# Early dense weights loaded sooner and rounded later, another order of the first loads and of TensorE's step

## The chip, the cores and the metric

The kernel runs on one core of one Trainium2 chip. The metric is the device time of one execution in microseconds (us), as the median of several runs.

## What is computed

Attention with buckets, and two dense blocks behind it. There are 2 x 8 heads of 768 positions and 64 features. A query sees a key only if six projected signs of both agree.

```python
mask = q_bucket[:, :, :, None] == k_bucket[:, :, None, :]
scores = np.where(mask, scale * q @ k.T, -1e9)
attn = softmax(scores)                       # over 768 keys
x = (attn @ v) gathered to 1536 x 512
h = x @ w_in;  g = P(h) / Q(h);  x = g @ w_out          # 512 -> 2048 -> 512
h = x @ w_in;  g = h * clip(h + 3, 0, 6) / 6;  out = g @ w_out
```

## The kernel before

Each engine has its own instruction stream, written out by hand with semaphores between them. The attention stage runs over 8 pairs of heads (`PAIRS`). A head has 6 tiles of 128 queries, so a pair has 12 steps, and tile n is number 12 i + j. I write "step 7" for j = 7. Step j of a pair contains, on each engine and in this order:

- TensorE (`step`, line 863): the scores of tile n into one of two banks; the turning (transposing) of the probabilities of tile n - 3, in two halves, by six transposes; in odd steps a third of a weighing of values by the probabilities of the pair before (`weigh`, line 824); at j = 1 the projection of the next pair (`project`). The scores of tile n wait for the exponential of tile n - 2 (line 808), since both use one bank. In the last pair the weighings stand at steps 1, 2, 4, 6, 8 and 9.
- VectorE (line 637): the maximum of tile n, the inverse of the row sum of n - 1, its copy of the turned second half of n - 3; at j = 2 the threshold that makes the bit rows of the next pair (line 595), at t = 1 of a head (t counts the tiles of a head) the lower halves of the head after next (line 603). The threshold writes the one tile `bits`, so it waits until the last head's bit rows have been moved out of it (line 599).
- GpSimd (line 404): scale and bias of tile n, the normalising of tile n - 1, and, a step behind ScalarE, the lower part of early weights.
- ScalarE (`step`, line 471): a copy of the weighed values at a head's start, the exponential of tile n - 1, at a head's start the upper halves of the head after next (`split_hi`), its copy of the turned first half of n - 3 (`take_turned`), and, in steps `EARLY_AT` of pairs 3 to 6, the rounding of one half of a dense weight slot (`split_weights`).

SyncE asks for nearly all DMAs, in one queue written by hand: raw heads, values, the moves that place keys and bit rows of a head in other partitions (`place_head`, line 289, with four waits inside it) and the weights (`load_weights`, line 301). In pairs 3 to 6 (`EARLY_PAIR`, four of them) it loads one dense slot each, w_in and w_out, 256 KB each, through the two buffers `w_raw`; a buffer is free again when GpSimd has subtracted from it.

Head 0 is loaded twice: straight into `raw[0][0]`, and with queries and keys exchanged into `raw[1][0]`, the tile that pair 1's first head needs next. Behind the attention stage the two dense blocks run over 3 chunks of 512 tokens and 16 slots each.

Of the kernel before, what the change touches and what calls it, by code (L numbers as in the profile page):

```python
# [24 lines left out]
ACT = mybir.ActivationFunctionType  # L25
AX = mybir.AxisListType

P = 128
# [5 lines left out]
def bucket_attention_and_two_mlps(nc, q, k, v, proj, w_in0, w_out0, poly_a, poly_b, w_in1, w_out1, out):  # L34
# [19 lines left out]
    TURN_LAG = 3  # L54
# [6 lines left out]

    EARLY_SLOTS = 4
    EARLY_PAIR = PAIRS - 1 - EARLY_SLOTS
    EARLY_AT = (4, 8)

    QC = 1.0 + 1e-6
    assert DM == HEADS * D and 2 * D == P and CHUNK == BANK and TILES == 6 and KT == 4
# [6 lines left out]
    def dram_head(i, u):  # L74
        return (i % BATCH) * HEADS + (i // BATCH) * 2 + u
# [15 lines left out]
    with ctx:  # L91
        def sb(name, shape, dt=F32, stack=ctx):
            return stack.enter_context(nc.sbuf_tensor(name, shape, dt))
# [33 lines left out]
        with attn:  # L127
            raw = [[sb(f"raw{e}{u}", [P, SEQ], F32, attn) for u in range(2)] for e in range(2)]
            pt_first = [[None, None], [None, None]]
            for g in range(2):  # L130
                pt_first[0][g] = sb(f"pt_first0{g}", [P, TILES, HALF], F32, attn)
            q_cross, k_cross, q_main, k_main = zip(*[
                [sb(f"{name}{u}", [P, SEQ], F32R, attn) for name in ("q_cross", "k_cross", "q_main", "k_main")]
                for u in range(SETS)])
            bits = sb("bits", [P, HALF], F32R, attn)
            v_nat = [[sb(f"v_nat{e}{u}", [P, TILES, D], F32, attn) for u in range(2)] for e in range(2)]
            probs = [sb(f"probs{j}", [P, SEQ], F32, attn) for j in range(4)]
            for g in range(2):
                pt_first[1][g] = sb(f"pt_first1{g}", [P, TILES, HALF], F32, attn)
            pt_second = [sb(f"pt_second{g}", [P, TILES, HALF], F32, attn) for g in range(2)]  # L140
            attn.pop_all().close()
        t_abs = [sb(f"t_abs{j}", [P, CHUNK]) for j in range(2)]
        t_den = [sb(f"t_den{j}", [P, CHUNK]) for j in range(2)]
# [112 lines left out]
        @block.sync  # L256
        def _(sp):
            def load_raw(i, u):
                to = raw[i % 2][u]
                sp.dma_start(to[0:D, :], q_dram[dram_head(i, u), :, :]).then_inc(raw_in[i % 2][u], 16)  # L260
                sp.dma_start(to[D:P, :], k_dram[dram_head(i, u), :, :]).then_inc(raw_in[i % 2][u], 16)

            def load_v(i):
                if i >= 2:
                    sp.wait_ge(pv_done, 2 * (i - 1))
                for u in range(2):
                    sp.dma_start(v_nat[i % 2][u][:, :, :].rearrange("p t d -> p (t d)"),
                                 v_dram[dram_head(i, u), :, :]).then_inc(v_in[i % 2], 16)

            def move(dst, src):  # L270
                return sp.dma_start(dst.bitcast(F32), src.bitcast(F32))

            def place_keys(h):

                c = h % SETS
                sp.wait_ge(hi_made, h + 1)
                move(k_main[c][0:D, :], q_main[c][D:P, :]).then_inc(moved_in[c], 16)
                move(k_cross[c][0:D, :], q_main[c][D:P, :]).then_inc(moved_in[c], 16)

            def place_bits(queue, h, side):  # L280

                c, at = h % SETS, 2 * QUAD * (h % 2) + MASKROWS * side
                to = (q_main, k_main)[side][c]
                for half in range(2):
                    cols = slice(HALF * half, HALF * (half + 1))
                    rows = slice(at + QUAD * half, at + QUAD * half + MASKROWS)
                    queue.dma_start(to[D:KROWS, cols].bitcast(F32), bits[rows, :].bitcast(F32)).then_inc(main_in[c], 16)  # L287

            def place_head(h):

                c = h % SETS
                place_keys(h)
                sp.wait_ge(bits_made, h // 2 + 2)
                place_bits(sp, h, 1)
                sp.wait_ge(lo_made, h + 1)
                move(k_cross[c][D:P, :], q_cross[c][D:P, :]).then_inc(moved_in[c], 16)
                sp.wait_ge(moved_in[c], moved(h))
                move(q_cross[c][D:P, :], q_main[c][0:D, :]).then_inc(main_in[c], 16)
                place_bits(sp, h, 0)

            def load_weights(m, f):

                at = FT * m + f
                for j, src in enumerate((w_in_dram[m][:, :, P * f:P * (f + 1)], w_out_dram[m][:, f, :])):
                    after(sp, w_lo_made, 2 * at - 1 + j)
                    dst = w_raw[j][:, :]
                    if j == 0:
                        dst = dst.rearrange("p (c n) -> p c n", c=KT)
                    sp.dma_start(dst, src).then_inc(w_in_sem[j], 16)

            sp.dma_start(raw[0][0][0:D, :], q_dram[dram_head(0, 0), :, :]).then_inc(raw_in[0][0], 16)
            sp.dma_start(raw[1][0][D:P, :], q_dram[dram_head(0, 0), :, :]).then_inc(swapped_in, 16)
            sp.dma_start(proj_raw[D:P, :], proj).then_inc(proj_in, 16)
            load_raw(0, 1)
            sp.wait_ge(bits_made, 1)
            sp.wait_ge(first_q, 2)
            place_bits(sp, 0, 0)
            load_v(0)
            place_head(1)
            sp.wait_ge(first_k, 2)  # L320
            load_raw(1, 0)
            load_raw(1, 1)
            load_raw(2, 0)
            load_raw(2, 1)
            sp.dma_start(a_col[:, :], poly_a.partition_broadcast(P)).then_inc(poly_in, 16)
            sp.dma_start(b_raw[:, :], poly_b.partition_broadcast(P)).then_inc(poly_in, 16)

            for h in range(NHEAD):
                i, u = divmod(h, 2)
                if u == 0 and i >= 1:  # L330
                    load_v(i)
                if h + 2 < NHEAD:
                    place_head(h + 2)
                if h + 6 < NHEAD:
                    load_raw((h + 6) // 2, h % 2)
                if u == 0 and EARLY_PAIR <= i < EARLY_PAIR + EARLY_SLOTS:
                    load_weights(0, i - EARLY_PAIR)
            for f in range(EARLY_SLOTS, FT):
                load_weights(0, f)
            for f in range(FT):  # L340
                load_weights(1, f)

            def store(c):

                for j in range(4):
                    sp.wait_ge(y_free, 4 * (CHUNKS + c) + 4 + j + 1)
                    tile = 4 * c + j
                    sp.dma_start(out_dram[tile // TILES, tile % TILES, :, :],
                                 (t_den + t_num)[j][:, :]).then_inc(stored[j], 16)

            for c in range(CHUNKS):
                store(c)
            for j in range(4):
                sp.wait_ge(stored[j], 16 * CHUNKS)
# [65 lines left out]
        @block.scalar  # L420
        def _(act):

            act.dma_start(raw[0][0][D:P, :], k_dram[dram_head(0, 0), :, :]).then_inc(raw_in[0][0], 16)
            act.dma_start(proj_raw[0:D, :], proj).then_inc(proj_in, 16)
            act.dma_start(raw[1][0][0:D, :], k_dram[dram_head(0, 0), :, :]).then_inc(swapped_in, 16)
            act.wait_ge(sel_made, 4)
            for c in range(2):
                act.dma_start(bit_col[:, c:c + 1], bit_row[0:1, c, :]).then_inc(bit_col_in, 16)
# [58 lines left out]

            act.wait_ge(swapped_in, 32)
            for to in (k_main, k_cross):
                nc.scalar.activation(to[0][0:D, :], raw[1][0][0:D, :], ACT.Copy).then_inc(first_k, 1)  # L490
            act.wait_ge(bits_made, 1)
            for half in range(2):
                cols, rows = slice(HALF * half, HALF * (half + 1)), QUAD * half + MASKROWS
# [92 lines left out]
        def _(dve):  # L586
# [72 lines left out]
            dve.wait_ge(bit_col_in, 32)  # L659
            threshold(0, slice(0, D), first=True)  # L660
            dve.wait_ge(swapped_in, 32)
            nc.vector.tensor_copy(q_cross[0][D:P, :], raw[1][0][D:P, :]).then_inc(first_q, 1)
            nc.vector.tensor_tensor(q_cross[0][0:D, :], raw[0][0][0:D, :], q_main[0][0:D, :].bitcast(F32),
                                    ALU.subtract).then_inc(first_q, 1)
            dve.wait_ge(first_q, 4)
# [117 lines left out]
        def _(pe):  # L783
# [79 lines left out]
            def step(i, j):  # L863
                u, t = divmod(j, TILES)
                h, n = 2 * i + u, 2 * TILES * i + j
                scores(h, i, u, n, j, t)
                if n >= TURN_LAG:
                    for half in range(2):
                        turn_probs(n - TURN_LAG, half)
                if i == PAIRS - 1 and j in LAST_WEIGH:  # L870
                    weigh(i - 1, *LAST_WEIGH[j])
                if 1 <= i < PAIRS - 1 and t in WEIGH_AT:
                    weigh(i - 1, u, WEIGH_AT[t])
                if j == PROJECT_AT and i + 1 < PAIRS:
                    project(i + 1, 0)
                    project(i + 1, 1)

            project(0, 0)
            project(0, 1)
# [87 lines left out]
```

## Time and profile before

| | |
|---|---|
| median of 3 runs | 822.86 us (822.78 to 823.11) |
| profiled execution | 823.14 us, its span 821.3 us |
| TensorE busy | 766.7 us, 93% of the span |
| VectorE, ScalarE, GpSimd busy | 479.0, 439.6, 223.3 us |
| the eight pairs' first scores at | 13.96, 49.85, 79.37, 108.38, 146.12, 183.85, 218.92, 255.36 us |
| dense blocks | from about 301 us to the end |
| moves of 192 KB between partitions, issue to landing | 2.6 us (keys and their lower halves) |

The span is the time from the first to the last instruction that the profile shows; the profiled execution's own time lies around it. A busy TensorE is not one at its peak: the length of a matmul in the rows is modelled and overlaps its neighbour's, so the distance from one start to the next is what counts. The granted clock (PEclk) is 1.00 at 2.4 GHz and 0.50 at 1.2 GHz; a mean between them is a mixture of the two.

### The profile page before, as it was taken

The numbers are of one execution on the slowest core, as the hardware profiler recorded it, in microseconds if no ns is written. First come the engines' busy times: TensorE is split into PE (matmuls) and PEld (weight loads), VectorE is DVE, ScalarE is ACT, GpSimd is POOL, SyncE is SP. The second block draws the span as 40 slices with busy tenths as digits, with TensorE's granted clock in tenths as the row PEclk, the third lists the DMA queues.
The fourth block names the chain that finished last, engine by engine and source line by source line (L and its number), as shares of the span: only waits on it lengthen the run. The fifth ranks groups of instructions, "written<-read, shape, count | busy, mean of one in ns | idle before, by whom it ended". The sixth has DMA issues, their size and how long they took to land.

```text
span 821.3 us, 11268 instructions
## 1 busy us (share of the span) xinstructions
PE 766.7 (93%) x3712; PEld 592.8 (72%) x3712; DVE 479.0 (58%) x793; ACT 439.6 (54%) x783; POOL 223.3 (27%) x364
## 2 busy tenths in 40 slices
PE   2689996887979999999999999999999999999998
PEld 1466665554656668888888888888888888888886
DVE  3577764555756668888988899984221322232223
ACT  1567665465656668987766689884222122212221
POOL 1455664554746514430000024443000000000000
PEclk9999997989989999999999999999999999999999
DMA  5634334333322013330000013331000100000001
GB/s 121 150 91 122 93 88 99 94 88 87 82 70 67 1 27 91 90 103 0 0 0 0 0 39 97 97 103 52 1 0 1 51 0 0 0 37 15 1 1 51
DMA packets 35372, 43.31 MB, mean 53 GB/s; under 512 B 4480, under 2 KB 23680, under 8 KB 35328
## 3 DMA queue, kind: packets, MB, share of 16 engines
q1 hardware_dynamic: 34752, 42.32, 19.4%
q10 hardware_dynamic: 576, 0.43, 0.2%
q8 instruction: 24, 0.39, 0.2%
q14 instruction: 20, 0.16, 0.1%
HBM read 26.61 MB, written 3.15 MB: 36 GB/s over the span
## 4 chain that ended last, share of the span: by engine, by line
PE 85%; DMA 4%; ACT 3%; SPq 3%; issue 2%; DVE 2%; ACTq 0%; POOL 0%; POOLq 0%; DVEq 0%
PE y_ps L912 32%; PE h_ps L858 11%; PE h_ps L859 11%; PE h_ps L860 11%; PE o_ps L838 6%; PE t_ps L821 6%; PE s_ps L811 4%; PE s_ps L812 3%; SPq L287 2%; DMA k_cross<-q_cross 2%; ACT probs L442 2%; DMA w_raw<-in_moe_w_in 2%; ACT q_main L436 1%; PE p_ps L795 1%; DMA bit_col<-bit_row 1%
## 5 line engine op out<-in xcount | busy, mean ns | idle before, releaser
L858 PE MATMUL h_ps<-x_hi,slot 128*128 (+1 forms) x384 | 149.7, 390 | 0.0
L859 PE MATMUL h_ps<-x_lo,slot 128*128 (+1 forms) x384 | 149.4, 389 | 0.0
L860 PE MATMUL h_ps<-x_hi,slot 128*128 (+1 forms) x384 | 149.4, 389 | 0.0
L704 DVE SCALAR_TENSOR_TENSOR t_abs<-t_abs,h_ps 128x512 f32<-128x512 f32 x48 | 33.0, 688 | 187.2 <-ACT t_abs L514 187.2
L401 POOL TENSOR_TENSOR slot<-w_raw,slot 128x512 fp32r<-128x512 f32 x64 | 81.8, 1295 | 206.9 <-ACT slot L469 206.7
L514 ACT ACTIVATE t_abs<-h_ps,three_col 128x512 f32<-128x512 f32 x48 | 33.1, 690 | 191.9 <-PE h_ps L860 191.9
L912 PE MATMUL y_ps<-g_hi,slot 128*128 128x512 f32 x384 | 126.1, 389 | 0.0
L442 ACT ACTIVATE probs<-s_ps,exp_bias,exp_scale 128x768 f32<-128x768 f32 x96 | 95.1, 991 | 52.0 <-POOL exp_bias L388 51.3
L612 DVE TENSOR_REDUCE neg_max<-s_ps 128x1 f32<-128x768 f32 x96 | 91.6, 954 | 52.6 <-PE s_ps L812 52.5
L912 PE MATMUL y_ps<-slot,g_hi 128*128 128x512 f32 x384 | 118.3, 389 | 0.0
L811 PE MATMUL s_ps<-k_cross,q_cross 128*128 128x512 f32 x192 | 79.6, 414 | 32.4 <-ACT probs L442 28.3
L394 POOL TENSOR_SCALAR probs<-probs,row_inv 128x768 f32<-128x768 f32 x96 | 95.2, 992 | 34.9 <-DVE row_inv L618 34.5
L821 PE MATMUL t_ps<-ident,probs 128*128 128x128 f32 x576 | 88.5, 287 | 4.1 <-ACT pt_second L453 2.3
L811 PEld LDWEIGHTS s_ps<-k_cross,q_cross 128*128 128x128 f32 x192 | 39.6, 206 | 69.9 <-issue 45.3
L858 PEld LDWEIGHTS h_ps<-x_hi,slot 128*128 128x128 f32 x384 | 72.1, 188 | 15.6 <-issue 0.6
L912 PEld LDWEIGHTS y_ps<-g_hi,slot 128*128 128x128 f32 x384 | 72.1, 188 | 15.3 <-DVE g_lo L710 0.2
L912 PEld LDWEIGHTS y_ps<-slot,g_hi 128*128 128x128 f32 x384 | 72.1, 188 | 14.9
L860 PEld LDWEIGHTS h_ps<-x_hi,slot 128*128 128x128 f32 x384 | 72.0, 188 | 14.9
L859 PEld LDWEIGHTS h_ps<-x_lo,slot 128*128 128x128 f32 x384 | 72.1, 188 | 14.8
L821 PEld LDWEIGHTS t_ps<-ident,probs 128*128 128x128 f32 x576 | 69.3, 147 | 11.2 <-issue 10.6
L912 PE MATMUL y_ps<-g_lo,slot 128*128 128x512 f32 x192 | 74.7, 389 | 0.0
L912 PE MATMUL y_ps<-slot,g_lo 128*128 128x512 f32 x192 | 74.7, 389 | 0.0
(71 smaller groups left out, 1173.0 us busy)
## 6 DMA issues: line engine op xcount, KB each, us to landing
w_raw<-in_moe_w_in SPq DMA_DIRECT2D x32, 256.0 KB, 2.7
w_raw<-in_moe_w_out SPq DMA_DIRECT2D x32, 256.0 KB, 2.7
raw<-in_q SPq DMA_DIRECT2D x17, 192.0 KB, 3.2
v_nat<-in_v SPq DMA_DIRECT2D x16, 192.0 KB, 2.5
raw<-in_k SPq DMA_DIRECT2D x15, 192.0 KB, 3.4
k_main<-q_main SPq DMA_DIRECT2D x15, 192.0 KB, 2.6
k_cross<-q_main SPq DMA_DIRECT2D x15, 192.0 KB, 3.1
k_cross<-q_cross SPq DMA_DIRECT2D x15, 192.0 KB, 2.6
```

The costliest lines, as they stand in the source:

```text
L394: nc.gpsimd.tensor_scalar(probs[j % 4][:, :], probs[j % 4][:, :], row_inv[:, r:r + 1], 1.0, ALU.mult, ALU.mult).then_inc(normed, 1)
L401: nc.gpsimd.tensor_tensor(slots[f][:, j, 1, :], w_raw[j][:, :], slots[f][:, j, 0, :].bitcast(F32), ALU.subtract).then_inc(w_lo_made, 1)
L442: nc.scalar.activation(probs[j % 4][:, :], s_ps[j % 2][:, 0:SEQ], ACT.Exp, scale=exp_scale[:, r:r + 1], bias=exp_bias[:, r:r + 1], accum_o ...
L514: nc.scalar.activation(t_abs[b][:, :], h_ps[b][:, :], ACT.Relu, bias=three_col[:, :])\
L612: nc.vector.tensor_reduce(neg_max[:, j % 4:j % 4 + 1], s_ps[j % 2][:, 0:SEQ], AX.X, ALU.max, negate=True)\
L811: mm(s_ps[j % 2][:, c0:c1], q_cross[c][:, rows], k_cross[c][:, c0:c1], start=True, stop=False)
L821: last = nc.tensor.transpose(t_ps[half][:, P * s:P * (s + 1)], probs[n % 4][:, c:c + P], ident[:, :])
L838: last = mm(weigh_bank(e)[D * u:D * (u + 1), 0:HALF], v_nat[i % 2][u][:, kt, :], pt(i, u, g)[:, kt, :], start=(kt == 0), stop=(kt == TILES ...
L858: mm(h_ps[b][:, :], w_hi, x_hi[:, kt, cols], start=(kt == 0), stop=False)
L859: mm(h_ps[b][:, :], w_hi, x_lo[:, kt, cols], start=False, stop=False)
L860: last = mm(h_ps[b][:, :], w_lo, x_hi[:, kt, cols], start=False, stop=(kt == KT - 1))
L912: last = mm(y_ps[d][:, :], still, moving, start=(f == 0 and a == 0), stop=(f == FT - 1 and a == 2))
```

## The change

Four things are edited:

1. The rounding of early weights moves from steps 4 and 8 to steps 7 and 10 of pairs 3 to 6 (`EARLY_AT`), on ScalarE and, a step later, on GpSimd.
2. SyncE asks for these weights at the start of the pair, behind the load of values, and no longer behind the placing of a head and a raw load.
3. The first loads: the projection first; head 0's exchanged copy goes into a probabilities buffer (`swapped`), so raw (1,0) is asked for at once; raw (1,1) comes before the placing of head 1, and the values of pair 0 behind it.
4. In TensorE's step the turning stands last, behind weighing and projection.

```diff
-    EARLY_AT = (4, 8)
+    EARLY_AT = (7, 10)
...
+            swapped = probs[3]
...
+            sp.dma_start(proj_raw[0:D, :], proj).then_inc(proj_in, 16)
             sp.dma_start(raw[0][0][0:D, :], q_dram[dram_head(0, 0), :, :]).then_inc(raw_in[0][0], 16)
-            sp.dma_start(raw[1][0][D:P, :], q_dram[dram_head(0, 0), :, :]).then_inc(swapped_in, 16)
-            sp.dma_start(proj_raw[D:P, :], proj).then_inc(proj_in, 16)
+            sp.dma_start(swapped[D:P, :], q_dram[dram_head(0, 0), :, :]).then_inc(swapped_in, 16)
             load_raw(0, 1)
+            load_raw(1, 0)
             sp.wait_ge(bits_made, 1)
             sp.wait_ge(first_q, 2)
             place_bits(sp, 0, 0)
+            load_raw(1, 1)
+            place_head(1)
             load_v(0)
-            place_head(1)
-            sp.wait_ge(first_k, 2)
-            load_raw(1, 0)
-            load_raw(1, 1)
             load_raw(2, 0)
             load_raw(2, 1)
...
                 if u == 0 and i >= 1:
                     load_v(i)
+                if u == 0 and EARLY_PAIR <= i < EARLY_PAIR + EARLY_SLOTS:
+                    load_weights(0, i - EARLY_PAIR)
                 if h + 2 < NHEAD:
                     place_head(h + 2)
                 if h + 6 < NHEAD:
                     load_raw((h + 6) // 2, h % 2)
-                if u == 0 and EARLY_PAIR <= i < EARLY_PAIR + EARLY_SLOTS:
-                    load_weights(0, i - EARLY_PAIR)
...
+            act.dma_start(proj_raw[D:P, :], proj).then_inc(proj_in, 16)
             act.dma_start(raw[0][0][D:P, :], k_dram[dram_head(0, 0), :, :]).then_inc(raw_in[0][0], 16)
-            act.dma_start(proj_raw[0:D, :], proj).then_inc(proj_in, 16)
-            act.dma_start(raw[1][0][0:D, :], k_dram[dram_head(0, 0), :, :]).then_inc(swapped_in, 16)
+            act.dma_start(swapped[0:D, :], k_dram[dram_head(0, 0), :, :]).then_inc(swapped_in, 16)
...
                 scores(h, i, u, n, j, t)
-                if n >= TURN_LAG:
-                    for half in range(2):
-                        turn_probs(n - TURN_LAG, half)
                 if i == PAIRS - 1 and j in LAST_WEIGH:
                     weigh(i - 1, *LAST_WEIGH[j])
                 if 1 <= i < PAIRS - 1 and t in WEIGH_AT:
                     weigh(i - 1, u, WEIGH_AT[t])
                 if j == PROJECT_AT and i + 1 < PAIRS:
                     project(i + 1, 0)
                     project(i + 1, 1)
+                if n >= TURN_LAG:
+                    for half in range(2):
+                        turn_probs(n - TURN_LAG, half)
```

The two readers of the exchanged copy read `swapped` instead of `raw[1][0]`.

## Rows read from the trace of the kernel before

**Rows 1.** Busy us of each engine in stretches, then clock, DMA share, GB/s

```profile
79.37:108.38 29.01, 28.56 (x178) 18.64 (x176) 21.24 (x42) 20.16 (x40) 17.82 (x37) 1.00 0.41 102
108.38:255.36 146.98, 121.89 (x706) 82.23 (x705) 85.28 (x165) 84.82 (x168) 81.36 (x153) 0.91 0.34 84
301.00:821.30 520.30, 517.02 (x2280) 427.45 (x2279) 297.92 (x447) 265.26 (x442) 71.53 (x56) 1.00 0.11 34
```

**Rows 2.** Waits in pairs 3 to 6: total us, times, longest

```profile
ACT slot L469 <- DMA w_raw<-in_moe_w_in: 28.2, 4, 7.9
```

**Rows 3.** The chain in pair 3: start us, us, what

```profile
113.51 0.78 PE p_ps L795 x8
...
124.92 3.45 DMA w_raw<-in_moe_w_in
```

**Rows 4.** Timeline of TensorE, the restart of pair 3: start us, us, what

```profile
130.14 0.77 PE L811 MATMUL s_ps<-k_cross,q_cross 128*128 128x512 f32 x1 [6.78 <-ACT probs L442]
```

**Rows 5.** Timeline of SyncE's DMA issues in pair 3

```profile
110.72 0.53 SPq L271 DMA_DIRECT2D k_main<-q_main  x1
...
117.34 0.79 SPq L287 DMA_DIRECT2D k_main<-bits  x1
```

**Rows 6.** Timeline of the first 27 us: bias of tile 0, issues, upper halves

```profile
17.22 0.27 POOL L388 TENSOR_SCALAR exp_bias<-neg_max,exp_scale 128x1 f32<-128x1 f32 x1 [0.20 <-POOL exp_scale L385]
...
18.77 1.59 SPq L287 DMA_DIRECT2D q_main<-bits  x2
20.40 0.52 SPq L260 DMA_DIRECT2D raw<-in_q  x1
...
24.37 0.84 ACT L436 ACTIVATE q_main<-raw 128x768 fp32r<-128x768 f32 x1 [11.64 <-DMA raw<-in_k]
```

**Rows 7.** Timelines of ScalarE and TensorE in pair 0 and after it

```profile
31.13 0.99 ACT L442 ACTIVATE probs<-s_ps,exp_bias,exp_scale 128x768 f32<-128x768 f32 x1 [3.97 <-POOL exp_bias L388]
...
52.55 0.48 ACT L453 ACTIVATE pt_second<-t_ps 128x384 f32<-128x384 f32 x1
52.99 0.99 ACT L442 ACTIVATE probs<-s_ps,exp_bias,exp_scale 128x768 f32<-128x768 f32 x1
...
32.26 0.50 PE L811 MATMUL s_ps<-k_cross,q_cross 128*128 128x512 f32 x1 [1.32 <-ACT probs L442]
...
36.38 0.47 PE L811 MATMUL s_ps<-k_cross,q_cross 128*128 128x512 f32 x1 [0.93 <-ACT probs L442]
```

**Rows 8.** Timelines of TensorE, ScalarE and VectorE in pair 2, tiles 8 to 10

```profile
99.33 0.50 PE L811 MATMUL s_ps<-k_cross,q_cross 128*128 128x512 f32 x1
...
100.14 0.82 PE L821 MATMUL t_ps<-ident,probs 128*128 128x128 f32 x6
100.71 0.48 PE L811 MATMUL s_ps<-k_cross,q_cross 128*128 128x512 f32 x1
...
103.85 0.50 PE L811 MATMUL s_ps<-k_cross,q_cross 128*128 128x512 f32 x1
...
100.66 0.49 ACT L453 ACTIVATE pt_first<-t_ps 128x384 f32<-128x384 f32 x1 [0.56 <-PE t_ps L821]
102.22 0.99 ACT L442 ACTIVATE probs<-s_ps,exp_bias,exp_scale 128x768 f32<-128x768 f32 x1 [1.06 <-POOL exp_bias L388]
...
100.33 0.96 DVE L612 TENSOR_REDUCE neg_max<-s_ps 128x1 f32<-128x768 f32 x1 [0.55 <-PE s_ps L812]
```

**Rows 9.** Groups of instructions in pairs 3 to 6: busy us, mean ns, idle before

```profile
L401 POOL TENSOR_TENSOR slot<-w_raw,slot 128x512 fp32r<-128x512 f32 x8 | 10.2, 1279 | 0.0
...
L607 DVE TENSOR_TENSOR q_cross<-raw,q_main 128x768 fp32r<-128x768 f32 x8 | 7.6, 951 | 0.0
...
L469 ACT ACTIVATE slot<-w_raw 128x512 fp32r<-128x512 f32 x8 | 5.0, 627 | 28.2 <-DMA w_raw<-in_moe_w_in 28.2
...
L600 DVE TENSOR_SCALAR bits<-p_ps,bit_col 128x384 fp32r<-128x384 f32 x4 | 2.7, 669 | 0.0
```

More of the change, by code:

```diff
@@ L489, in _ @@
             for to in (k_main, k_cross):
-                nc.scalar.activation(to[0][0:D, :], raw[1][0][0:D, :], ACT.Copy).then_inc(first_k, 1)
+                nc.scalar.activation(to[0][0:D, :], swapped[0:D, :], ACT.Copy).then_inc(first_k, 1)
             act.wait_ge(bits_made, 1)
@@ L661, in _ @@
             dve.wait_ge(swapped_in, 32)
-            nc.vector.tensor_copy(q_cross[0][D:P, :], raw[1][0][D:P, :]).then_inc(first_q, 1)
+            nc.vector.tensor_copy(q_cross[0][D:P, :], swapped[D:P, :]).then_inc(first_q, 1)
             nc.vector.tensor_tensor(q_cross[0][0:D, :], raw[0][0][0:D, :], q_main[0][0:D, :].bitcast(F32),
```

## Prediction

> **What bounds the kernel now.** I read the page first: TensorE is busy for 93% of the span, so a gain must come from the rest, or from TensorE's own waits. The stretches by stage show where these lie. From 301 us to the end, in the two dense blocks, TensorE works 517.02 of 520.30 us [rows 1]; the change touches nothing there. In the attention stage, pair 2 takes 29.01 us with TensorE busy 28.56; the four pairs 3 to 6, which also round early dense weights, take 146.98 us with 121.89 busy and a mean granted clock of 0.91 [rows 1]. Four plain pairs would take 4 x 29.01 = 116.04, so the early weights cost 30.94 us. The waits of that stretch name the cause: ScalarE sits 28.2 us, four times, in front of a rounding whose weights have not landed [rows 2]. The chain shows the way: the weights are asked for at 124.92 and land 3.45 us later [rows 3], while ScalarE came to the rounding at its step 4; the exponentials queue behind it, the scores behind them, and TensorE then restarts slowly after 6.78 us of idle: its first scores matmul takes 0.77 us [rows 4], the one of 99.33 takes 0.50 [rows 8].
>
> The second hole is at the start. The bias of tile 0 is ready at 17.22 + 0.27 = 17.49 [rows 6], but ScalarE first has to take the upper halves of head 2, whose raw tile is asked for at 20.40 and lands at 24.37 (11.64 us of idle) [rows 6]. Only then come the exponentials.
>
> **The change, part by part.**
>
> *First loads.* The swapped copies go to a probabilities buffer, so raw tile (1,0) is free and is asked for right behind (0,1), at about 4 us by four issues of 0.6 us. Its two loads move 0.39 MB in front of nothing that is awaited before 9 us. The projection goes first; its dependants are then blocked by the bit columns as before, so I book nothing. Head 2 is then ready when ScalarE comes to it at 12.7, and the first exponential starts at 17.5. Next limits, from here: exponential start to dependent score start is 32.26 - 31.13 = 1.13 us [rows 7]; maximum start to its exponential's start is 102.22 - 100.33 = 1.89 us [rows 8]. Score 2 could start at 18.6; TensorE is also occupied by the projections of pair 1 there, so I take 19.6. VectorE then comes to the threshold of pair 1, which must wait until head 1's bit rows have left the shared tile: their two issues start at 18.77 and take 1.59 in sum [rows 6], and with 2 to 3.4 us to land (2 is an estimate, under the 2.6 us that the page gives for moves of 192 KB; 3.4 is the wait for raw (1,0) behind its second issue) that is 22.4 to 23.8. Taking 22.4: threshold 0.67 [rows 9], maximum 3 at 23.1, exponential 3 at 25.0, its copy behind it and exponential 4 at 26.5 (0.99 and 0.5 more), score 6 at 27.6. The path by scores 2 and 4 gives the same 27.6 (2 x (1.0 + 1.89 + 1.13) from 19.6). It started at 36.38 [rows 7]. **Gain 8.8 us**, and from there on the pair runs as before, bound by latency. Bounds: 7.4 with the later landing; 9.8 if both paths come a microsecond earlier.
>
> *SyncE's order in early pairs.* The two weight loads now follow the load of values directly, which is issued at the pair's start (108.38), so the weights are asked for at about 109.4 and are there by 113. They are taken at steps 7 and 10 (about 125 and 132 in old time). The wait of 28.2 us is gone with a cover of 10 us. Behind the weights in the queue stand the key moves, which started at 110.72 [rows 5] after waiting for head 8's upper halves; two issues of 0.6 us end at 110.7, so they are hardly late, and what follows them waits for the bits of the next pair until 117.34 anyway [rows 5]: 6 us of cover. From the second early pair on, the load of weights also waits for GpSimd's subtraction of the pair before, which will end some 2 us into the pair, still ahead of the keys. Cost nothing; without that cover it would be at most the 2 us.
>
> *Order in TensorE's step.* Two tiles take 103.85 - 99.33 = 4.52 us, all of it TensorE work: scores to scores 100.71 - 99.33 = 1.38 in the step without weighing, of which score to turn is 0.81 and turn to score 0.57; the rest is the step with weighing [rows 8]. The new order does the same work, so by TensorE alone nothing changes: the turn of the odd step starts at 4.52 - 0.57 = 3.95. But ScalarE works in order: it copies this turn before it takes the exponential of the same tile, on which the scores two tiles later wait. That path is: turn to copy 100.66 - 100.14 = 0.52 [rows 8], copy to exponential 52.99 - 52.55 = 0.44 and exponential to scores 1.13 [rows 7], together 2.09, against 1.95 of TensorE work (0.57 + 0.81 + 0.57). So each pair of tiles becomes a loop of 0.52 + 0.44 + 1.13 + (3.95 - 1.38) = 4.66 us, 0.14 longer. Bounds: nothing, if the copy starts earlier behind a weighing; 0.3 if it takes 0.16 more. At a head's start an x copy stands between, of the same 128x384 and so 0.44 us: 5.10. The projection adds 0.78 to one [rows 3].
>
> One more edge: VectorE does its own copy and the lower halves (0.95 us [rows 9]) after the late turn, and only then the next maximum. Counted from turn 1: turn 0.82 and copy 0.5, lower halves to 2.3, maximum 2 from there; in the first head of a pair copy 0.55 and threshold 0.67 follow, so maximum 3 is at 4.5 and its exponential at 6.4, against 4.66 + 0.96 = 5.6 by the loop. I take 0.7 once a pair (bounds 0 and 0.9). A pair is then (5.10 + 0.78) + 4.66 + (4.66 + 0.7) in its first head and 5.10 + 4.66 + 4.66 in its second: **30.3 instead of 29.01**. Pairs 1 and 2: +2.6. The last pair has four weighings before a step without one: +0.6.
>
> *Rounding at steps 7 and 10.* The old splits lay beside the stall; now they lie in the loop. ScalarE's is 0.627 us [rows 9]: at step 7 it stands before exponential 7, which the loop waits for (about 0.55 with overlap); at step 10 the exponential has 1 us of spare. GpSimd's is 1.279 us [rows 9] and comes between the bias of tile 8 and that of tile 9: counted from turn 7, bias 8 and the normalising end at 5.0, the subtraction at 6.3, exponential 9 starts at 7.0, against 6.2 with ScalarE's delay: 0.85. Together **1.4 a pair** (bounds 0.5 and 2.2). At step 10 it ends beside the wait for the next maximum.
>
> *Sum.* Pairs 3 to 6: 4 x (30.3 + 1.4) = 126.8, against 146.98: -20.2. Start -8.8, pairs 1 and 2 +2.6, last pair +0.6: -25.8. The profiled execution took 823.14 us, 1.84 around its span of 821.3; it gives 797.3. The median of the runs, 822.86, lies 0.28 below: **797.1 us**.
>
> **The rivals.**
>
> *The order costs nothing, or gives what waits in front of turns there are.* If ScalarE's and VectorE's copies fit, pairs stay at 29.01: -8.8 - 146.98 + 4 x (29.01 + 1.4) = -34.1: 788.7 us. For it: only 0.14 us decides. Against it: every row of the path is measured, and the old exponentials have little spare.
>
> *The loop is longer.* 0.3 us for a two-tile loop instead of 0.14 (some 40 loops, +6), or the start gives only 7.4 and an early pair costs 2.2: 803 to 806 us.
>
> *Slower than before, by the clock.* The new order makes TensorE pause in every loop. If the clock falls to its level of 1.2 GHz there, the same work takes twice as long; the first scores of [rows 4] and [rows 8] (0.77 against 0.50, each with a fixed part) show the sign of it. With 25.8 us to give back, it decides from 52 us of wall time at the lower level on, two of the seven pairs; all seven would add about 190 us. I price a case at four pairs, 60 us of full-speed time becoming 120: 857 us. Against it: pair 2 has pauses too, and its mean granted clock is 1.00 [rows 1]; the slow restarts in pairs 3 to 6 follow long idle times, 6.78 us the first [rows 4]. The Trainium skill ("TensorE: Matmul & The Clock Gate", section "A second HAM failure mode: psum-queue depth-cycling") says that small pauses between groups of matmuls, in each turn of a loop, can make the clock go up and down; by that rule the time would lie on this side. The trace of pair 2, at 1.00 with 0.45 us of pauses, does not agree with it.
>
> *The weights are late still, or the wait moves to SyncE.* If the stall of the early pairs stayed whole, only the start would gain: 814 us plus the order's 6 = 817. The 10 us of cover speak against it.
>
> **How the numbers follow.** Forecast 0.48, own range 792 to 801; order free 0.24; longer loop 0.20; stall stays 0.04; clock 0.03; 0.01 for anything else. The range from 785 to 806 leaves out the last ones and the tails. Faster by over 0.2% (what a measurement of this kernel can tell from no change): 0.96; within it 0.01; slower 0.03.
>
> **What would show it.** Right: no idle before ScalarE's rounding of early weights; pairs 3 to 6 at 31 to 32 us each and at a granted clock near 1.00; pairs 1 and 2 at 30 to 30.6; exponential 0 at 17.5 and score 6 at 27 to 29; the dense stage unchanged at 520 us. Wrong: pairs 1 and 2 at 29.0 or less (the order is free), or above 31; a wait of the scores for head 2 or 3; a clock below 0.95 in pairs 1 to 6.

## The result, and the profile after

The changed kernel takes 789.01 us (median of 4 runs, 787.94 to 790.67) against 822.99 us for the kernel before beside it: ratio 0.9589, 95% interval 0.9569 to 0.9609. That is 8.1 us below the forecast of 797.1, inside the range, and at the place of the rival "the order costs nothing" (788.7). The profiled execution took 787.94 us, its span is 786.1.

Stretches of the changed kernel, as in [rows 1]: pair 1, pair 2, pairs 3 to 6, the rest, and of it the dense stage.

```profile
41.05:69.81 28.76, 28.19 (x176) 18.69 (x177) 21.25 (x41) 19.29 (x40) 16.71 (x38) 1.00 0.49 122
69.81:99.01 29.20, 28.41 (x179) 18.72 (x178) 21.70 (x41) 19.78 (x41) 16.39 (x37) 1.00 0.41 100
99.01:220.73 121.72, 113.66 (x707) 74.70 (x706) 87.13 (x164) 83.23 (x169) 74.16 (x152) 1.00 0.40 102
220.73:786.10 565.37, 560.41 (x2541) 455.74 (x2539) 327.63 (x502) 294.32 (x500) 90.68 (x95) 1.00 0.11 33
265.90:786.10 520.20, 516.92 (x2280) 427.42 (x2278) 297.96 (x447) 265.11 (x442) 71.43 (x56) 1.00 0.11 34
```

| stretch | before | forecast | after |
|---|---|---|---|
| pair 0 ends at | 49.85 | 41.05 | 41.05 |
| pair 1 | 29.52 | 30.8 | 28.76 |
| pair 2 | 29.01 | 30.3 | 29.20 |
| pairs 3 to 6 | 146.98 | 126.8 | 121.72 |
| last pair and all behind it | 565.94 | 566.5 | 565.37 |

Both gains are there: 8.80 us at the start, where 8.8 were forecast, and 25.26 us in pairs 3 to 6, where 20.2 were. What missed is the price of the new order: a plain pair (one that rounds no weights) was to go from 29.0 to 30.3, and pair 2 takes 29.20. In pair 1 another 0.7 us comes on top, and it isn't the order's: its first step, scores 0 to scores 1, took 2.12 us before, in a stretch whose granted clock was 0.66 (49 to 51 us), and takes 1.45 now (1.44 with the old order, in "all but the order"). The granted clock of the changed kernel is 1.00 in all stretches.

The waits of pairs 3 to 6, as in [rows 2], have no line for the weights any more. These are waits of ScalarE and TensorE in the loop now (us in total, times, longest):

```profile
ACT probs L442 <- POOL exp_bias L388: 15.8, 16, 1.7
...
ACT pt_second L453 <- PE t_ps L821: 12.7, 13, 1.6
...
PE s_ps L811 <- ACT probs L442: 8.1, 20, 0.8
...
ACT probs L442 <- PE t_ps L821: 3.4, 4, 0.9
```

The first microseconds, as in [rows 6], from the timelines of the changed kernel by engine:

```profile
3.91 0.60 SPq L261 DMA_DIRECT2D raw<-in_q  x1
...
9.38 0.67 DVE L600 TENSOR_SCALAR bits<-p_ps,bit_col 64x384 fp32r<-64x384 f32 x1 [2.32 <-DMA bit_col<-bit_row]
...
12.56 1.58 ACT L436 ACTIVATE q_main<-raw 128x768 fp32r<-128x768 f32 x2 [2.94 <-DVE bits L600]
...
15.34 0.76 PE L811 MATMUL s_ps<-k_cross,q_cross 128*128 128x512 f32 x1 [4.87 <-DMA k_main<-bits]
...
18.59 0.27 POOL L388 TENSOR_SCALAR exp_bias<-neg_max,exp_scale 128x1 f32<-128x1 f32 x1 [0.20 <-POOL exp_scale L385]
18.89 0.99 ACT L442 ACTIVATE probs<-s_ps,exp_bias,exp_scale 128x768 f32<-128x768 f32 x1 [4.75 <-POOL exp_bias L388]
...
22.34 0.68 DVE L600 TENSOR_SCALAR bits<-p_ps,bit_col 128x384 fp32r<-128x384 f32 x1 [0.26 <-DMA q_main<-bits]
```

ScalarE has head 2's upper halves behind it by 14.1 us instead of 25.2 (two copies from 12.56), and the first exponential is held by its bias alone. The forecast booked nothing for the new order of the first loads; but the bit columns come at 9.38, against 8.71 before, and the first scores at 15.34, against 13.96. VectorE's threshold does wait for the bit rows (0.26 us, at 22.34), as the sum had it (22.4), and the exponential of tile 3 behind it starts at 24.80 (25.0 in the sum). The exponential of tile 4 waits for its own late scores and starts at 26.97 instead of 26.5.

The loop in pair 2, tiles 10 and 11, as in [rows 8]: scores, turn, scores, weighing, turn, scores.

```profile
94.49 0.51 PE L811 MATMUL s_ps<-k_cross,q_cross 128*128 128x512 f32 x1
...
95.32 0.82 PE L821 MATMUL t_ps<-ident,probs 128*128 128x128 f32 x6
96.03 0.50 PE L811 MATMUL s_ps<-k_cross,q_cross 128*128 128x512 f32 x1
...
96.94 0.54 PE L838 MATMUL o_ps<-pt_first,v_nat 128*64 128x384 f32 x1
...
98.38 0.87 PE L821 MATMUL t_ps<-ident,probs 128*128 128x128 f32 x6
99.01 0.47 PE L811 MATMUL s_ps<-k_cross,q_cross 128*128 128x512 f32 x1
```

And the same neighbours in the kernel before, in pair 2: scores at 100.71 [rows 8], then the turn, the weighing, and the next scores at 103.85 [rows 8].

```profile
101.51 0.97 PE L821 MATMUL t_ps<-ident,probs 128*128 128x128 f32 x6
102.41 0.54 PE L838 MATMUL o_ps<-pt_first,v_nat 128*64 128x384 f32 x1
```

Read by starts, a step with weighing was 0.80 (scores to turn) + 0.90 (turn to weighing) + 1.44 (weighing to scores) = 3.14 us. It is now 0.91 (scores to weighing) + 1.44 (weighing to turn) + 0.63 (turn to scores) = 2.98.

Nearly all of the 0.16 us was a wait, and not work. The second half of a turn waits for VectorE's copy of the turn before (`turn_probs`), and that copy was still running:

```profile
101.28 0.54 DVE L628 COPY pt_first<-t_ps 128x384 f32<-128x384 f32 x1
```

It ends at 101.82. Of the six transposes that start at 101.51, the first three follow each other after 0.11 us; the fourth starts at 101.96, 0.23 us behind the third, and the fifth 0.14 behind that. The pause is too short for the timeline to print. Without it the hand-over from turn to weighing takes 0.75 to 0.78 us (0.77 at 97.11 in this kernel), so TensorE's own work was 0.80 + 0.75 + 1.44 = 2.99 us, the same as the 2.98 of now. In pair 2 of the kernel before, three of the six steps with weighing hold this wait (at 87.39, 101.51 and 106.05), and one holds a third of it (92.02). The prediction's sentence "the new order does the same work" was right. "All of it TensorE work" was not: 0.15 us of the 4.52 were this wait, and in the new order a weighing stands between the two turns and covers it.

### The profile page after: what moved, and what is told of

It reads as the page before. It is cut to its first block, busy times and chain, and to the rows that moved or that the text cites. A ratio compares the mean times of both kernels' runs of the same rounds, so it can differ in the third digit from the quotient of the medians.

```text
span 786.1 us, 11268 instructions
## 1 busy us (share of the span) xinstructions
PE 753.8 (96%) x3712; PEld 583.2 (74%) x3712; DVE 482.2 (61%) x793; ACT 436.9 (56%) x783; POOL 214.8 (27%) x364
## 3 DMA queue, kind: packets, MB, share of 16 engines
HBM read 26.61 MB, written 3.15 MB: 38 GB/s over the span
## 4 chain that ended last, share of the span: by engine, by line
PE 89%; ACT 4%; issue 3%; DVE 2%; DMA 1%; ACTq 1%; POOL 0%; POOLq 0%
PE y_ps L912 33%; PE h_ps L860 11%; PE h_ps L858 11%; PE h_ps L859 11%; PE o_ps L838 8%; PE t_ps L821 5%; PE s_ps L811 5%; PE s_ps L812 3%; ACT probs L442 3%; ACT x_hi L460 1%; DMA bit_col<-bit_row 1%; DVE neg_max L612 1%; PE p_ps L795 1%; PE p_ps L838 1%; DMA k_main<-bits 0%
## 5 line engine op out<-in xcount | busy, mean ns | idle before, releaser
L811 PE MATMUL s_ps<-k_cross,q_cross 128*128 128x512 f32 x192 | 75.0, 391 | 20.4 <-ACT probs L442 15.5
L394 POOL TENSOR_SCALAR probs<-probs,row_inv 128x768 f32<-128x768 f32 x96 | 88.4, 921 | 1.4 <-DVE row_inv L618 1.0
L821 PEld LDWEIGHTS t_ps<-ident,probs 128*128 128x128 f32 x576 | 63.7, 140 | 27.7 <-issue 14.2
L821 PE MATMUL t_ps<-ident,probs 128*128 128x128 f32 x576 | 81.3, 277 | 1.1 <-ACT pt_second L453 0.9
L838 PE MATMUL o_ps<-pt_first,v_nat 128*64 128x384 f32 x180 | 67.3, 498 | 0.0
```

What stands on the lines that cost most here:

```text
L394: nc.gpsimd.tensor_scalar(probs[j % 4][:, :], probs[j % 4][:, :], row_inv[:, r:r + 1], 1.0, ALU.mult, ALU.mult).then_inc(normed, 1)
L811: mm(s_ps[j % 2][:, c0:c1], q_cross[c][:, rows], k_cross[c][:, c0:c1], start=True, stop=False)
L821: last = nc.tensor.transpose(t_ps[half][:, P * s:P * (s + 1)], probs[n % 4][:, c:c + P], ident[:, :])
L838: last = mm(weigh_bank(e)[D * u:D * (u + 1), 0:HALF], v_nat[i % 2][u][:, kt, :], pt(i, u, g)[:, kt, :], start=(kt == 0), stop=(kt == TILES ...
```

## The experiments

Each was timed beside the kernel before on the same chip; the chips differ between groups of rows, so kernels are best compared by their ratios. Plain pair is pair 2, early pairs are 3 to 6 together, both by the profile of that run.

| kernel | median us | ratio to before (95%) | plain pair | early pairs |
|---|---|---|---|---|
| changed kernel | 789.01 | 0.9589 (0.9569 to 0.9609) | 29.20 | 121.72 |
| order only | 822.28 | 1.0001 (0.9989 to 1.0012) | 29.15 | 148.54 |
| weights only | 795.20 | 0.9675 (0.9658 to 0.9692) | 29.02 | 119.08 |
| first loads only | 814.84 | 0.9907 (0.989 to 0.9925) | 29.02 | 145.75 |
| all but the order | 786.96 | 0.9572 (0.9555 to 0.959) | 29.01 | 119.06 |
| later steps only | 794.94 | 0.968 (0.9664 to 0.9696) | 29.03 | 119.12 |
| asked sooner only | 792.11 | 0.9643 (0.9626 to 0.9659) | 29.03 | 116.10 |
| raw behind bits | 790.24 | 0.9625 (0.9609 to 0.9642) | 29.16 | 121.67 |
| raw before projection | 788.25 | 0.9594 (0.9578 to 0.961) | 29.16 | 121.66 |
| change, even steps | 784.21 | 0.9532 (0.9518 to 0.9547) | 29.17 | 116.66 |
| change, weighing first | 802.47 | 0.9757 (0.9742 to 0.9772) | 31.62 | 126.83 |
| change, split later | 787.05 | 0.9564 (0.955 to 0.9579) | 28.72 | 119.44 |
| old order, even steps | 784.10 | 0.9539 (0.9525 to 0.9554) | 29.02 | 116.06 |

### The parts alone

**Order only.** The kernel before with

```diff
                 scores(h, i, u, n, j, t)
-                (turn_probs of n - TURN_LAG)
                 (weigh, project)
+                (turn_probs of n - TURN_LAG)
```

> The kernel before with the new order of TensorE's step alone. Theory of the prediction (loop): TensorE's work is the same, each pair becomes 30.3 us instead of 29.0 by the path turn, copy, exponential, scores; pairs 1 and 2 near 30.3, the total 5 to 8 us longer, 828 to 831. Theory formed on the trace after (shorter step): a step with weighing needs 2.98 us of TensorE instead of 3.14, since the drain between turning and weighing goes, and the waits at a head's start and behind the threshold give it back; pair 2 at 29.2, the total within 2 us of before, 821 to 825.

The ratio is 1.0001. Pair 2 takes 29.15 us, and the last pair with all behind it 565.26 against 565.94:

```profile
79.55:108.70 29.15, 28.34 (x180) 18.69 (x178) 21.72 (x41) 19.72 (x41) 16.37 (x37) 1.00 0.40 98
257.24:822.50 565.26, 560.31 (x2541) 455.78 (x2539) 327.43 (x502) 294.44 (x500) 89.67 (x95) 1.00 0.11 33
```

Both theories had a loss per pair; the loss is 0.14 us, not 1.3, and the last pair, which mixes steps otherwise, gains 0.7. The number of the theory "shorter step" stands: 2.98 us instead of 3.14. Its reason doesn't: what went was the wait for VectorE's copy, as shown above. Other waits, at a head's start and behind VectorE's lower halves, cost a little more than that gives.

**Weights only.** The kernel before with `EARLY_AT = (7, 10)` and `load_weights` ahead of `place_head`.

> The kernel before with the early weights asked for sooner and rounded at steps 7 and 10, everything else as before. If the rounding costs in the loop as much in the old order (1.2 us a pair in the trace after), pairs 3 to 6 take 4 x 30.2 = 121 us instead of 147 and the total is 797. If the old order hides it, pairs take 29.0 to 29.5 and the total is 793 to 794. If the stall needs the other edits to go, 810 or more.

Early pairs take 119.08 us, 29.77 each: the old order hides ScalarE's part of the rounding and not GpSimd's, 0.75 a pair, where the new order pays 30.43 - 29.20 = 1.23.

**First loads only.** The kernel before with item 3 of the change.

> The kernel before with the new first loads alone. The prediction's sum: 8.8 us less, 814.2. Rival: the gain at the start is given back in the unchanged pairs, since a pair's start does not move the end when a DMA paces it: 818 or more. The trace after shows the first pair 8.8 us earlier at its end.

The kernel takes 814.84 us against 822.11 beside it, 7.3 us less where 8.8 were expected; nothing is given back behind pair 0. In this profile pair 1 starts at 43.25 instead of 41.05. Of these 2.2 us, 0.4 lie ahead of the first scores, 0.7 between scores 0 and 4, and 1.1 behind, where some steps run slowly: the scores of tile 4 take 0.79 us here, and 0.50 in the changed kernel.

```profile
25.18 0.79 PE L811 MATMUL s_ps<-k_cross,q_cross 128*128 128x512 f32 x1 [0.50 <-ACT probs L442]
```

```profile
24.07 0.50 PE L811 MATMUL s_ps<-k_cross,q_cross 128*128 128x512 f32 x1 [1.14 <-ACT probs L442]
```

Slow matmuls are not all of it. Pair 0 takes 26.96 us in the next kernel, whose scores of pair 0 from tile 4 on take 0.47 to 0.50 each, and 25.71 in the changed kernel. Most of this difference is the step from scores 9 to scores 10: 3.79 us there and 3.80 in the kernel before, but 2.92 in the changed kernel. In that step VectorE's lower halves and GpSimd's normalising meet. In the kernel before, and then in the changed kernel:

```profile
40.73 0.91 POOL L394 TENSOR_SCALAR probs<-probs,row_inv 128x768 f32<-128x768 f32 x1
40.90 1.54 DVE L607 TENSOR_TENSOR q_cross<-raw,q_main 128x768 fp32r<-128x768 f32 x1
```

```profile
32.71 0.95 DVE L607 TENSOR_TENSOR q_cross<-raw,q_main 128x768 fp32r<-128x768 f32 x1
32.80 1.62 POOL L394 TENSOR_SCALAR probs<-probs,row_inv 128x768 f32<-128x768 f32 x1
```

The one that starts second is the long one. The maximum of tile 8 stands behind the lower halves, so in the first case the scores wait longer. The eight profiles whose lower halves take 1.54 us here all show 3.79 or 3.80 for this step, and the other six 1.97 to 2.92. Which case comes depends on which of the two starts first, and they start 0.1 to 0.2 us apart.

**All but the order.** The changed kernel with the old order of the step.

> The changed kernel with the old order of TensorE's step. Theory of the prediction (the order costs 1.3 us a pair): about 9 us faster than the changed kernel, 780. Theory formed on the trace after: within 2 us of the changed kernel, 787 to 791, with plain pairs at 29.0 and early pairs at 30 to 30.5.

Faster than the changed kernel by its ratio (0.9572 against 0.9589), by about 1.4 us, with intervals that overlap: by the medians alone the order's cost is not shown. The stretches behind pair 0 are sharper: pair 2 at 29.01 against 29.20, early pairs at 119.06 against 121.72, the last pair and all behind it at 565.86 against 565.37. In sum the order costs this kernel some 2.3 us behind pair 0, most of it (1.9) where it meets the rounding; the profile's pair 0 goes the other way by 1.2, and other kernels of either order show pair 0 anywhere from 25.71 to 27.66. The ratios of the three parts multiply to 0.9586, and 0.9589 was measured. So the parts add within intervals of 0.001 to 0.002 to either side, which are too wide to show the 1.9 us.

```profile
71.07:100.08 29.01, 28.57 (x178) 18.62 (x177) 21.22 (x42) 20.13 (x40) 17.76 (x37) 1.00 0.41 102
100.08:219.14 119.06, 114.72 (x707) 74.69 (x705) 85.40 (x165) 83.39 (x168) 79.77 (x152) 1.00 0.41 103
219.14:785.00 565.86, 561.16 (x2540) 455.75 (x2538) 326.05 (x501) 294.29 (x499) 90.55 (x95) 1.00 0.11 33
```

### The two edits for the weights

**Later steps only.** The kernel before with `EARLY_AT = (7, 10)`.

> The kernel before with the rounding at steps 7 and 10 alone; the weights are asked for as late as before. If the later step gives most of the cover, the weights (asked for some 16.5 us into a pair, there 3.5 us later) come about 3 us after step 7 has need of them: a stall of 1 to 4 us in place of 7 to 8, pairs 3 to 6 at 31 to 34 us, total 800 to 812. If asking sooner is what counts, pairs stay above 35 and the total above 815.

Early pairs 119.12, as good as with both edits. My estimate of a stall of 1 to 4 us was too dear: the weights land at 128.5 in pair 3 and ScalarE waits 1.12 us for them at step 7, the longer of two such waits (1.9 us in all four pairs, against 28.2 before). The pairs are no longer for it.

```profile
128.56 0.63 ACT L469 ACTIVATE slot<-w_raw 128x512 fp32r<-128x512 f32 x1 [1.12 <-DMA w_raw<-in_moe_w_in]
```

**Asked sooner only.** The kernel before with

```diff
                     load_v(i)
+                if u == 0 and EARLY_PAIR <= i < EARLY_PAIR + EARLY_SLOTS:
+                    load_weights(0, i - EARLY_PAIR)
                 if h + 2 < NHEAD:
...
-                if u == 0 and EARLY_PAIR <= i < EARLY_PAIR + EARLY_SLOTS:
-                    load_weights(0, i - EARLY_PAIR)
```

> The kernel before with the weights asked for at the pair's start alone, rounded at steps 4 and 8 as before. In even steps the next exponential has over 1 us to spare. Theory (only the step's parity prices the rounding): pairs 3 to 6 at 29.0 to 29.4 instead of 29.77 with steps 7 and 10, total 792 to 794. Rival (each rounding costs its GpSimd and ScalarE time wherever it stands): 29.8 or more, 795. If the weights are late at step 4 (they ask 1 us into the pair, step 4 comes 12 us in), a stall shows before the rounding.

Early pairs take 116.10 us, 29.03 each, which is the plain pair: here the early weights cost nothing at all. Either edit alone removes the stall; moving the rounding on top of asking sooner is no gain but a loss of 0.75 us a pair. Why shows in the timelines of the odd step 7 in the changed kernel:

```profile
119.39 0.62 ACT L469 ACTIVATE slot<-w_raw 128x512 fp32r<-128x512 f32 x1
119.91 0.98 ACT L442 ACTIVATE probs<-s_ps,exp_bias,exp_scale 128x768 f32<-128x768 f32 x1
...
122.47 0.91 POOL L394 TENSOR_SCALAR probs<-probs,row_inv 128x768 f32<-128x768 f32 x1
123.34 1.27 POOL L401 TENSOR_TENSOR slot<-w_raw,slot 128x512 fp32r<-128x512 f32 x1
124.59 0.22 POOL L385 TENSOR_SCALAR exp_scale<-neg_max 128x1 f32<-128x1 f32 x1
...
126.45 0.50 PE L811 MATMUL s_ps<-k_cross,q_cross 128*128 128x512 f32 x1 [0.82 <-ACT probs L442]
```

ScalarE's rounding stands between a copy and the exponential that gates the scores. GpSimd's subtraction (1.27 us) stands ahead of the bias of tile 9, and TensorE waits 0.82 us for the exponential behind it. At step 8 of the kernel that asks sooner only, the same subtraction ends where the next maximum would have kept GpSimd waiting, 0.16 us from it:

```profile
130.12 0.62 ACT L469 ACTIVATE slot<-w_raw 128x512 fp32r<-128x512 f32 x1
131.28 0.99 ACT L442 ACTIVATE probs<-s_ps,exp_bias,exp_scale 128x768 f32<-128x768 f32 x1 [0.54 <-POOL exp_bias L388]
...
133.64 1.29 POOL L401 TENSOR_TENSOR slot<-w_raw,slot 128x512 fp32r<-128x512 f32 x1
135.09 0.23 POOL L385 TENSOR_SCALAR exp_scale<-neg_max 128x1 f32<-128x1 f32 x1 [0.16 <-DVE neg_max L612]
```

**Change, even steps.** The changed kernel with `EARLY_AT = (4, 8)`.

> The changed kernel with the rounding back at steps 4 and 8, weights still asked for at the pair's start. Theory (the odd step's exponential and bias gate the loop, an even step's do not): pairs 3 to 6 from 30.43 to 29.2 to 29.5, total about 4 us less than the changed kernel, 784 to 786. Rival (in the new order, with the turn late, each rounding costs): 30 or more.

116.66 us, 29.17 each, the plain pair of the new order. The rival falls. In either order the rounding is free at steps 4 and 8 and costs at step 7; at step 10 it is free too, since the two steps behind it stay at 2.98 and 1.85 us. That is one odd step against three even ones.

### The order, the hand-over and VectorE

**Change, weighing first.** The changed kernel with weigh and project ahead of the scores.

> The changed kernel with TensorE's step in the order weigh and project, scores, turn. Theory (the 0.16 us that the new order saves per weighing is the drain between a turn and a weighing): turn and weighing are neighbours again, so a two-tile round needs 4.5 us of TensorE again; but here the scores come 1.4 us later against the exponentials, so the path decides: plain pairs at 30 or more. If the drain theory is wrong, the distance from one start to the next around a weighing stays 2.98 in sum.

Plain pair 31.62 us; the path decides, as expected. A new wait adds to it: the first weighing of a head now comes before VectorE has taken the last lower halves.

```profile
87.00 0.82 PE L821 MATMUL t_ps<-ident,probs 128*128 128x128 f32 x6
87.75 0.54 PE L838 MATMUL o_ps<-pt_first,v_nat 128*64 128x384 f32 x1
...
93.88 0.54 PE L838 MATMUL o_ps<-pt_first,v_nat 128*64 128x384 f32 x1 [1.52 <-DVE x_lo L634]
```

It also settles where the 0.16 us come from. The turn at 82.08 hands over to the weighing after 0.90 us and the one at 87.00 after 0.75. In the first, VectorE's copy of the turn before ends at 82.39 and the fourth transpose starts at 82.53, 0.23 us behind the third; in the second all six follow each other after 0.11. So 0.15 us is that wait, and it comes and goes with VectorE's copy. What is left between neighbours is this: a weighing starts 0.20 us behind the last transpose, scores start 0.03 us behind it. Why was not tested apart.

**Change, split later.** VectorE's lower halves at tile 3 of a head:

```diff
-                if t == 1 and h + 2 < NHEAD:
+                if t == (1 if i == 0 else 3) and h + 2 < NHEAD:
                     split_lo(h + 2)
```

> The changed kernel with VectorE's lower halves at tile 3 of a head instead of tile 1 (pair 0 as before). Theory of the prediction (they hold maximum 2, and with the threshold maximum 3): the step from scores 4 to scores 5 in the first head falls from 1.98 to about 1.5, a plain pair from 29.20 to 28.7 to 28.9. Rival: it is the threshold alone, or the late turn; then 1.9 or more stays, and the pair stays at 29.2. Danger: the moves of the next heads start 4.5 us later; if they are late a wait for them shows at a head's start.

Scores 4 to scores 5 in the first head falls from 1.98 to 1.55 us and the plain pair from 29.20 to 28.72, the best one seen:

```profile
71.96:100.68 28.72, 28.31 (x176) 18.70 (x177) 21.79 (x42) 19.71 (x41) 16.40 (x36) 1.00 0.42 103
100.68:220.12 119.44, 114.39 (x705) 74.85 (x705) 89.93 (x166) 83.29 (x169) 74.09 (x151) 1.00 0.42 106
```

So the edge on VectorE that the prediction named is real: the maximum stands behind the lower halves. It also acted in the second head, where the prediction had none: scores 9 to scores 10 falls from 3.15 to 2.98. Part of it is paid again (scores 5 to the next head's first scores take 3.52 instead of 2.99). No wait for the moves appears. Not combined with the even steps.

### The start

**Raw behind bits** and **raw before projection**, the changed kernel with one load moved each:

```diff
             load_raw(0, 1)
-            load_raw(1, 0)
             (waits, place_bits(sp, 0, 0))
+            load_raw(1, 0)
```

```diff
-            (proj_raw, raw[0][0], swapped)   on SyncE;  (proj_raw, raw[0][0]) on ScalarE
+            (raw[0][0], swapped, proj_raw)   on SyncE;  (raw[0][0], proj_raw) on ScalarE
```

> The changed kernel with raw (1,0) asked for behind the first placing of bit rows instead of ahead of it. Theory A (its 0.39 MB delay the bit columns and the bit rows): first scores at 14.0 to 14.5 us instead of 15.3, first exponential still held by its bias at 17.5 to 18, total about 1 us less, 788. Theory B (the projection's two slow small loads in front of the raw data delay everything): first scores stay at 15.2 or later.

> The changed kernel with the raw halves of head 0 asked for first and the projection third and second, as before the change. Theory B: first scores at 14.0 to 14.6 us, total about 1 us less. Theory A (see the kernel with raw (1,0) behind the bits): first scores stay at 15.2 to 15.4.

The first scores start at 15.13 and 15.23 us, both held by the bit rows, as in the changed kernel (15.34). So neither load alone is the cause of the 1.4 us. They have two halves. The bit columns come 0.7 us later, at 9.38 against 8.71, and stay late in both kernels here (9.24 and 9.43); that half stays open, and moving both loads back at once was not run. The other 0.7 us lies behind: from the end of the second issue to the first scores it is 2.9 us in the changed kernel (10.08 + 2.38 to 15.34) and 2.2 before (9.41 + 2.37 to 13.96). What differs there in all three kernels is what shares the DMA engines with the bit rows, a raw load where there was a load of values. That is an observation; putting the values in front of raw (1,1) was not run. In total raw behind bits missed its expected 788 us and is slower than the changed kernel by its ratio, with intervals that just touch; pair 0 alone took 1.9 us longer in its profile (27.62 against 25.71).

### The best of both

**Old order, even steps.** First loads and asking sooner from the change; order and steps from before.

> First loads and asking sooner from the change, TensorE's order and steps 4 and 8 from before. Sum of the parts measured alone: pairs 3 to 6 at 29.03 each, last pair as before, start some 7 to 8 us earlier: 783.5 to 785, about 4 us faster than the changed kernel. If the parts do not add (DMAs of the start and of the weights collide, or the rounding needs the new order), 787 or more.

784.10 us, ratio 0.9539 (0.9525 to 0.9554), below the changed kernel (0.9589) and all but the order (0.9572), and level with the changed kernel at even steps (0.9532, 0.9518 to 0.9547). The sum of the parts (783.5 to 785) holds.

## Why the prediction came out as it did

**First loads, 8.8 us.** The profile after shows 8.80, but by luck. Score 6 was forecast at 27.6 and started at 28.20, held up by first scores that came 1.4 us late, an effect booked at nothing. The rest of pair 0, which was to run as before, then took 12.85 us instead of 13.47, because its step from scores 9 to scores 10 fell to 2.92 us from 3.80, as shown under "first loads only". Alone, the edit gives 7.3 us, just under the lower bound of 7.4; in the profiles of the other kernels with this edit and the scores first in the step, pair 0 ends at 41.56 to 43.25.

**SyncE's order, nothing.** Right: the key moves of pair 3 start 2.56 us into the pair, against 2.34 before, and no wait for weights or heads appears. What the sum did not see is that the edit was enough by itself; the prediction treated "sooner" and "later" as one edit, and half of it was a cost.

**TensorE's order, 1.3 us a pair: the term that was mis-sized.** It measured 0.14 to 0.19. The path turn, copy, exponential, scores exists and is as long as worked out: at 89.23 to 91.34 in the changed kernel 0.59 + 0.39 + 1.13 = 2.11 us, forecast 2.09. But the loop also holds the stretch from scores through weighing to the turn, taken as 3.95 - 1.38 = 2.57; it is 0.91 + 1.44 = 2.35. The 0.22 us too much are 0.16, nearly all of it the wait for VectorE's copy that had been counted as TensorE's work, and 0.06, because a turn behind a weighing hands over to scores after 0.63 us and not 0.57.

So the loop is 2.11 + 2.35 = 4.46 us and not 4.66. It runs from the scores of an odd tile to those of the next odd tile, and read that way pair 2 bears out nearly every term of the sum:

| from scores to scores | measured | booked, less 0.20 | what is on top of the loop |
|---|---|---|---|
| 11 to 1 | 4.83 | 4.90 | x copy, 0.37 (0.44 booked) |
| 1 to 3 | 5.24 | 5.24 | projection, 0.78 |
| 3 to 5 | 5.13 | 5.16 | VectorE's edge, 0.67 (0.7 booked) |
| 5 to 7 | 4.84 | 4.90 | x copy, 0.38 (0.44 booked) |
| 7 to 9 | 4.46 | 4.46 | nothing |
| 9 to 11 | 4.69 | 4.46 | VectorE's edge in the second head, 0.23 (nothing booked) |

The booked terms give 29.1 us, and the pair takes 29.2. In the kernel before, the same distances are 4.78, 5.59, 4.62, 4.69, 4.81 and 4.53 us. So the new order gains 0.35 at 1 to 3 and again at 7 to 9, loses 0.51 and 0.16 at the two loops with VectorE's edge, and 0.2 in sum at the heads' starts: 0.2 us longer. With the lower halves moved, the edge goes and the pair takes 28.72.

**Rounding at steps 7 and 10, 1.4 us a pair.** Measured 1.23: 0.50 for ScalarE (0.55 booked) and the rest for GpSimd. The mechanism and its place were right.

**The rivals.** "The order costs nothing" gave 788.7 and is nearest in number and in cause, though the order is not free: it trades one wait for others, and loses by about 2.3 us behind pair 0 in this combination. It was given 0.24; the reason that I gave against it, that each row of the path was measured, did not cover the stretch through the weighing, which was a difference of two sums and held a hidden wait. By the prediction's own signs the new order's price was wrong: pairs 1 and 2 came in at 28.76 and 29.20, beside the mark for a free order (29.0 or less) and far under the one for its being right (30 to 30.6). The clock did not fall: the changed kernel shows 1.00 in all stretches, with pauses in each loop. The Trainium skill ("TensorE: Matmul & The Clock Gate", section "A second HAM failure mode: psum-queue depth-cycling") warns of such pauses; at 0.2 to 0.8 us, once a few steps, this case shows none of it.

## What to carry to other kernels

When a stall has two independent cures, measure each alone: here the second one on top cost 0.75 us a pair and gave nothing. Before moving side work within a software pipeline, find which of its steps gate the loop (here the odd step 7, on ScalarE and, a step later, on GpSimd) and put it in the others, where 0.6 and 1.3 us of work were free. When the order of an engine's groups changes, look first at the starts within each group of the old order: a distance longer than its like can hold a wait of 0.1 to 0.2 us that no view prints, and it need not move along. The distance between each new pair of neighbours has to be bounded too.

## What the runs showed of the hardware

- Hand-over between groups on TensorE, start to start: turn to scores 0.57 us, or 0.63 when the turn stands behind a weighing; turn to weighing 0.75 to 0.78, and 0.90 where the turn itself waits for VectorE; scores to turn 0.80, scores to weighing 0.91. The two orders of a step sum up to nearly the same, 2.99 and 2.98 us.
- When VectorE's lower halves and GpSimd's normalising overlap, the one that starts second is longer: 1.54 us instead of 0.95 for the lower halves (at 40.90 in the kernel before), 1.62 instead of 0.91 for the normalising (at 32.80 in the changed kernel). No experiment set this apart.
- Pair 0 varies: 25.71 us in the changed kernel's profile, 27.62 and 26.33 in the two kernels that differ from it by one load. At the start matmuls can run slowly (a 512-column scores matmul of 0.79 us against 0.50, at 25.18 in the kernel with the first loads only), while the granted clock of that stretch reads 1.00. Later in pair 0 of the kernel before, the same length goes with a low clock: 0.80 us at 47.27, where the granted clock is 0.50 (47 to 49 us). The variation of pair 0 is of the size of the 2.7 us between the fastest and the slowest run of the changed kernel; what decides it was not tested.
